# A pipeline over batches from token mixing on, with the feed-forward in four chunks of 386 columns

## The chip, the cores and the metric

The kernel runs on one core of a Trainium2 chip. The metric is the device time of one execution in microseconds (us). The kernel before took 497.8, 505.08 and 505.54 us in three runs, a median of 505.08 us.

## The reference

Three layers run one after another; everything is float32. B = 2, H = 8, S = 768, D = 64, so C = H*D = 512, and F = 1024.

```python
# 1. attention: keep = the first n_global=8 keys, or 0 <= i-j < n_local=96; a bias by distance and head
a = softmax(where(keep, q @ k.T / 8 + bias, -1e9));  x = concat_heads(a @ v)          # [B, S, 512]
# 2. mixing
theta = x @ w_theta                                   # "angles"
zr, zi = x * cos(theta), x * sin(theta)
u = x + w_tok_r @ zr + w_tok_i @ zi                   # token mixing, over S, for each batch
v = u + relu(u @ w_ch)                                # channel mixing
# 3. feed-forward
h = relu(v @ w_in)                                    # [B, S, 1024]
g = h * sigmoid(conv3_over_tokens(h, conv_w))         # tap weights per column, zero padded
out = g @ w_out                                       # [B, S, 512]
```

Token mixing needs all six 128-row tiles of z of its own batch and none of the other batch. The convolution needs one neighbour row on either side.

## The kernel before

Tokens are handled in tiles of 128 rows: NT = 6 per batch, TT = 12 in all. From the angles on, every product is made of three matmuls: each float32 operand is held as a high part (type float32r, made by a copy) and a low part (the float32 value less the high part), and `product` (L373) adds high*high, high*low and low*high into one PSUM bank. So each operand costs a copy, mostly on ACT, and a subtraction, on DVE or POOL. Every engine runs its own list in the order in which it is written; semaphores are the only link between them.

- **Attention** (`banded`, on each engine): 48 units, one for a pair of heads and a tile of queries. PE computes scores, transposed probabilities and the weighted values; ACT takes exponentials and copies; DVE takes maxima (`minus_maxima`, L786), makes the bias tables of the first units (L827) and divides. Meanwhile POOL splits w_theta (L312 and L313), later w_ch and the first rows of w_tok, for which SP issues the loads.
- **Angles** (loops at L493, L635, L932 and L344): for each of 12 tiles PE transposes x and multiplies by w_theta, ACT copies the high part and rounds theta/2pi (L643), DVE makes the low part (L928), reduces the angle in three steps (L938, L942, L945) and clamps it (L948), ACT takes abs, sin and cos (L651, L652, L655), DVE makes x*cos (L957), POOL makes x*sin (L347), ACT copies the high part of both (L661) and POOL makes the two low parts (L351, L353). `r` and the others are double buffered.
- **Token mixing** (L510): 12 groups of 36 matmuls in the order of `MIXES` (L195), both batches side by side, so that each of the six row blocks of w_tok is loaded and split once (`load_w_tok`, L223; `high_rows`, L614; `low_rows`, L918). All of z, for both batches, is 96 KB per partition. DVE adds y to x (L974).
- **Channel mixing** (L525): four chunks of 384 tokens by four blocks of output columns, 12 matmuls each. u is transposed on PE ahead of its use (`transpose_u`, L478), split on ACT (L676) and DVE (L966); v is made on DVE (L994, L1001), copied on ACT (L681) and its low part made on DVE (L981). ACT and POOL split w_in (L696, L358) and w_out (L700, L362) between.
- **Feed-forward** (L542): for each batch, for each of FB = 8 blocks of 128 hidden columns, PE makes h in two halves of 384 tokens (24 matmuls); then relu (L712) and the first tap (L717) on ACT, two taps on DVE (L1017, L1020), sigmoid on ACT (L724), the gate product on DVE (L1027), the high part of g on ACT (L731) and its low part on POOL (L367), all of these over 768 tokens at a time. Behind the eight blocks PE makes the 6 output tiles of the batch, 144 matmuls (L566), ACT copies them out (L750) and SP stores them.

Before the feed-forward of a batch starts, everything ahead of it has ended for both batches. In the feed-forward ACT's and DVE's lists are ordered so:

```python
ACT:  relu(n)  first_tap(n)  sigmoid(n-1)  high_g(n-2)      # relu(n) waits for gate(n-2)
DVE:  conv(n)  gate(n-1)
POOL: low part of g(n-2)
```

Of the kernel before, what the change touches and what calls it, by code (L numbers as in the profile page):

```python
# [29 lines left out]
def build(nc, q, k, v, qk_laid, v_laid, n_global, n_local, w_theta, w_tok, w_ch, w_in, conv_w, w_out, out):  # L30
# [20 lines left out]
    with ctx:  # L51
# [15 lines left out]
        x_flat = x[:].rearrange("p t c -> p (t c)")  # L67
        wch = at("wch", [P, 2, CB, C], F32R, 25)
        wth = at("wth", [P, 2, CB, C], F32R, 41)
        wrows = at("wrows", [P, 2, 2 * NT, P], F32, 57)  # L70
        wraw = at("wraw", [P, CB, C], F32, 69)
        winraw = at("winraw", [P, 2, F], F32, 69)
# [3 lines left out]
        def att(name, shape, dt):  # L76
# [22 lines left out]
        assert a0 <= 207, a0  # L99
# [23 lines left out]
        z = at("z", [P, TT, 2, 2, C], F32R, 77)  # L123
        xT = at("xT", [P, 2, 2, CB * P], F32R, 173)
        th_k = at("th_k", [P, C], F32, 181)
        th_r = at("th_r", [P, 2, C], F32, 183)
        trig = at("trig", [P, 2, 2, C], F32, 187)
        zf = at("zf", [P, 2, 2, C], F32, 69)

        wT = [at("wT0", [P, 2, 2 * NT, P], F32R, 195), at("wT1", [P, 2, 2 * NT, P], F32R, 173)]  # L130

        vT = at("vT", [P, 2, CB, B * S], F32R, 77)
        win = at("win", [P, 2, CB, F], F32R, 125)
        uT = [at("uT0", [P, 2, CB, HALF], F32R, 41), at("uT1", [P, 2, CB, HALF], F32R, 57)]
        vtmp = at("vtmp", [P, 2, HALF], F32, 53)
        g = at("g", [P, 2, FB, S], F32R, 1)
        h_sb = at("h_sb", [P, 2, S + 2], F32, 49)
        cv = at("cv", [P, 2, S], F32, 55.5)
        sg = at("sg", [P, 2, S], F32, 61.5)
        gf = at("gf", [P, 2, S], F32, 67.5)  # L140
        wout = at("wout", [P, 2, FB, C], F32R, 157)
        ob = at("ob", [P, 2, C], F32, 189)
        woutraw = at("woutraw", [P, 4, C], F32, 193)
# [6 lines left out]
            x_all taps_in ident_ready consts_in mask_step bias_ready peak_ready qk_in0 qk_in1 v_in0 v_in1  # L150
            scores_ready max_ready probs_ready pt_ready pt_copied o_ready den_ready rec_ready x_done wraw_in wth_step
            wth_ready wch_ready xt_ready x_hi x_lo theta_ready theta_read k_ready turns_ready r_step r_ready
# [20 lines left out]

        S_BANK = [psum[:, 0:2, :], psum[:, 2:4, :]]
        PT_BANK = [bank[4], bank[5]]
        O_BANK = [bank[6], bank[7]]

        def pair(p):
            return p // HP, 2 * (p % HP)
# [898 lines left out]
```

## Time and profile before

| | |
|---|---|
| median of three runs | 505.08 us (497.8 to 505.54) |
| the profiled execution | 506.55 us, of which its span is 504.8 us |
| PE busy | 439.5 us, 87% of the span |
| DVE, ACT, POOL busy | 281.3, 200.7, 130.5 us |
| granted PE clock, mean | 0.938 of full speed |
| the chain that ended last | PE 55%, DVE 28%, ACT 7%, issue 6%, POOL 2% |
| DMA | 27.46 MB, 54 GB/s over the span |

The span runs from the first to the last instruction of the profiled execution; 1.75 us of that execution's time lie around it. PE's busy time counts matmuls that overlap, so it says where PE had work and not that it ran at its peak. "Granted clock" is the share of full speed that PE's clock was given: 1.00 is 2.4 GHz and 0.50 is 1.2 GHz, and a value between is a mean over a stretch that had both.

### The profile page before, as it was taken

To read this page: it belongs to the slowest core of one execution; us is meant where nothing else is said; L and a number is where in the kernel's file an instruction comes from. 1 tells how busy PE (TensorE), PEld (TensorE's weight loads), DVE (VectorE), ACT (ScalarE), POOL (GpSimd) and SP (SyncE) were. 2 spreads that over 40 slices of the span, in tenths; PEclk is the share of its full clock that TensorE was granted. 3 is DMA by queue.
4 is the path that set the end of the run, shared out by engine and by line. 5 is a ranking of instruction groups with operands and counts; after the bars stand their busy time and mean duration, and the time that the engine had idled before them with its cause. 6 is when DMAs were issued, how large, how long until landed. Compare 5 with 4: busy or idle time off the path is not lost.

```text
span 504.8 us, 6172 instructions
## 1 busy us (share of the span) xinstructions
PE 439.5 (87%) x2352; PEld 374.8 (74%) x2352; DVE 281.3 (56%) x474; ACT 200.7 (40%) x360; POOL 130.5 (26%) x86
## 2 busy tenths in 40 slices
PE   1699999998885677499999999778897999996997
PEld 0488888887764556388888888778897878996875
DVE  5845666669289999502222114879667640266620
ACT  1334666664176656401011003333455541455531
POOL 1500000008037678800000000444413340023340
PEclk9857999998599889889999999889899999999999
DMA  7414333350100000101300002130000002100012
GB/s 288 175 66 130 128 129 130 130 149 16 49 0 1 1 1 1 34 28 64 145 1 0 0 1 83 43 125 1 1 2 0 1 0 83 43 0 1 0 43 84
DMA packets 11119, 27.46 MB, mean 54 GB/s; under 512 B 4176, under 2 KB 4176, under 8 KB 11088
## 3 DMA queue, kind: packets, MB, share of 16 engines
q1 hardware_dynamic: 11088, 27.05, 15.6%
q8 instruction: 19, 0.31, 0.2%
q14 instruction: 12, 0.10, 0.1%
HBM read 23.90 MB, written 3.15 MB: 54 GB/s over the span
## 4 chain that ended last, share of the span: by engine, by line
PE 55%; DVE 28%; ACT 7%; issue 6%; POOL 2%; DMA 1%; DVEq 0%; SPq 0%; ACTq 0%
PE bank L379 27%; PE bank L428 8%; PE bank L566 7%; DVE gf L1027 7%; PE bank L395 6%; PE bank L413 4%; PE bank L400 3%; DVE cv L1017 3%; ACT cv L717 3%; DVE zf L957 3%; ACT h_sb L712 2%; DVE vtmp L1001 2%; DVE th_r L945 2%; DVE th_k L938 1%; DVE th_r L942 1%
## 5 line engine op out<-in xcount | busy, mean ns | idle before, releaser
L379 PE MATMUL bank<-z,wT 128*128 128x512 f32 x432 | 101.9, 397 | 6.9 <-DVE wT L921 6.9
L379 PEld LDWEIGHTS bank<-z,wT 128*128 128x128 f32 x432 | 82.5, 192 | 24.5 <-DVE wT L921 7.3
L379 PE MATMUL bank<-vT,win 128*128 128x384 f32 x384 | 69.7, 341 | 9.7 <-ACT h_sb L712 7.8
L379 PEld LDWEIGHTS bank<-vT,win 128*128 128x128 f32 x384 | 68.0, 192 | 11.3 <-ACT h_sb L712 9.1
L566 PE MATMUL bank<-wout,g 128*128 128x512 f32 x288 | 66.3, 390 | 1.2 <-POOL g L367 1.2
L566 PEld LDWEIGHTS bank<-wout,g 128*128 128x128 f32 x288 | 53.8, 188 | 13.2 <-POOL g L367 2.2
L367 POOL TENSOR_TENSOR g<-gf,g 128x768 fp32r<-128x768 f32 x16 | 34.4, 2154 | 92.4 <-ACT g L731 92.4
L379 PE MATMUL bank<-wth,xT 128*128 128x512 f32 x144 | 42.0, 447 | 18.2 <-DVE xT L928 18.2
L428 PE MATMUL bank<-v_sb,pT 128*128 128x65 f32 x352 | 51.1, 293 | 0.0
L379 PEld LDWEIGHTS bank<-wth,xT 128*128 128x128 f32 x144 | 30.0, 215 | 27.7 <-DVE xT L928 21.2
L428 PEld LDWEIGHTS bank<-v_sb,pT 128*128 128x128 f32 x352 | 49.9, 218 | 0.0
L974 DVE TENSOR_TENSOR x<-bank,x 128x512 f32<-128x512 f32 x12 | 8.3, 690 | 73.5 <-PE bank L379 73.5
L1017 DVE SCALAR_TENSOR_TENSOR cv<-h_sb,convw,cv 128x768 f32<-128x768 f32 x16 | 16.3, 1018 | 55.0 <-ACT cv L717 55.0
L395 PE MATMUL bank<-qk_sb 64*128 64x232 f32 (+1 forms) x192 | 34.6, 442 | 13.4 <-DMA qk_sb<-qk_laid 6.9
L580 ACT ACTIVATE pr<-bank,small 128x232 f32<-128x232 f32 (+1 forms) x96 | 36.7, 437 | 21.4 <-DVE small L786 21.2
L591 ACT ACTIVATE pT<-bank 128x512 f32<-128x512 f32 (+1 forms) x48 | 26.9, 561 | 38.8 <-PE bank L413 38.7
L358 POOL TENSOR_TENSOR win<-winraw,win 128x1024 fp32r<-128x1024 f32 x4 | 9.5, 2380 | 124.9 <-ACT win L696 124.9
L379 PE MATMUL bank<-uT,wch 128*128 128x384 f32 x192 | 38.9, 359 | 1.6 <-DVE vtmp L994 1.6
L379 PEld LDWEIGHTS bank<-uT,wch 128*128 128x128 f32 x192 | 35.7, 202 | 1.9 <-DVE vtmp L994 1.9
L1027 DVE TENSOR_TENSOR gf<-h_sb,sg 128x768 f32<-128x768 f32 x16 | 34.8, 2187 | 0.1
L780 DVE TENSOR_REDUCE small<-bank 128x2 f32<-128x464 f32 (+1 forms) x48 | 29.0, 604 | 10.5 <-PE bank L400 10.5
L712 ACT ACTIVATE h_sb<-bank 128x384 f32<-128x384 f32 x32 | 14.4, 490 | 45.8 <-DVE gf L1027 35.2
(87 smaller groups left out, 546.9 us busy)
## 6 DMA issues: line engine op xcount, KB each, us to landing
qk_sb<-qk_laid SPq DMA_DIRECT2D x8, 792.0 KB, 4.5
v_sb<-v_laid SPq DMA_DIRECT2D x8, 780.0 KB, 4.5
wrows<-w_tok_laid SPq DMA_DIRECT2D x6, 768.0 KB, 4.4
out<-ob SPq DMA_DIRECT2D x12, 256.0 KB, 2.1
winraw<-w_in_in SPq DMA_DIRECT2D x4, 512.0 KB, 4.3
woutraw<-w_out_in SPq DMA_DIRECT2D x8, 256.0 KB, 3.9
wraw<-w_theta_in SPq DMA_DIRECT2D x1, 1024.0 KB, 11.3
wraw<-w_ch_in SPq DMA_DIRECT2D x1, 1024.0 KB, 6.7
```

Of the source, the lines that this page charges most:

```text
L367: pool.tensor_tensor(g[:, 1, n % FB, :], gf[:, n % 2, :], g[:, 0, n % FB, :].bitcast(F32), ALU.subtract)\
L379: last = pe.matmul(dst, w[a], m[b], start=(i == 0 and j == 0), stop=(i == n - 1 and j == 2))
L395: pe.matmul(S_BANK[u % 2][:, h, cols], qk_sb[rows, pp, i * P:(i + 1) * P], qk_sb[rows, pp, S + c0:S + c1], start=True, stop=False)
L413: last = pe.transpose(PT_BANK[u % 2][:, slot * P:(slot + 1) * P], pr[:, u % 2, h, cols], ident[:])
L428: last = pe.matmul(O_BANK[u % 2][:, h * OW:(h + 1) * OW], pT[:, u % 2, slot * P:(slot + 1) * P], v_sb[:, pp, i, chunk, h, :], start=(chunk ...
L566: last = pe.matmul(OUT_BANK[t % 4][:], g[:, hi, f, i * P:(i + 1) * P], wout[:, lo, f, :], start=(f == 0 and j == 0), stop=(f == FB - 1 and ...
L580: last = act.activation(pr[:, u % 2, h, cols], S_BANK[u % 2][:, h, cols], ACT.Exp, bias=small[:, u % 2, 2 + h:3 + h], scale=SCALE)
L591: act.activation(d, src, ACT.Copy).then_inc(pt_copied, 1)
L712: act.activation(h_sb[:, n % 2, 1 + half * HALF:1 + (half + 1) * HALF], H_BANK[n % 2][half][:, 0:HALF], ACT.Relu).then_inc(h_relu, 1)
L780: dve.tensor_reduce(small[:, u % 2, 0:2], S_BANK[u % 2][:, :, cols], AX.X, ALU.max).then_inc(peak_ready, 1)
L1017: dve.scalar_tensor_tensor(out=c, in0=h[:, 1:S + 1], scalar=convw[:, 1, f:f + 1], in1=c, op0=ALU.mult, op1=ALU.add).then_inc(conv_step, 1)
L1027: dve.tensor_tensor(gf[:, m % 2, :], h_sb[:, m % 2, 1:S + 1], sg[:, m % 2, :], ALU.mult).then_inc(g_ready, 1)
```

## The change

The attention's program stays. From the angles on:

- **Angles**: the 12 tiles still come in one row, but sine, cosine and z follow at once only for batch 0 (tiles 0 to 5). Those of batch 1 are made on ACT, DVE and POOL while PE mixes the tokens of batch 0; `th_r` therefore holds six tiles. The clamp moves from DVE to POOL; x*cos and x*sin become one DVE instruction of 1024 columns (`weigh`), the two low parts of z one POOL instruction (`low_z`). PE transposes tile t+1, and ACT and DVE split tile t+2, ahead of the angle of tile t. PE no longer waits for all of x at once.
- **Weights**: POOL splits the first two row blocks of w_tok early instead of w_ch and one block; ACT and POOL split w_ch after the angles. The row blocks of w_tok are loaded and split once for each batch: 12 loads instead of 6.
- **Token and channel mixing**: six groups of batch 0, then those of batch 1 with the channel mixing of batch 0 between them. uT has one buffer instead of two; the low part of v moves from DVE to POOL.
- **Feed-forward**: 4 chunks by 8 blocks, n = 0 to 31, of HC = 386 columns on PE (two of them neighbour rows) and 384 or 386 on the other engines. The first chunk is made between channel-mixing products of batch 1; from then on PE alternates `hidden` of chunk c and `output` of chunk c-1. `ob` has three buffers.

The core of the diff (the lists of PE whole, of the others what the prediction speaks of):

```diff
 @@ SP
-            sp.wait_ge(wth_ready, 1)
-            sp.dma_start(wraw[:], w_ch...)
+            load_w_tok(2)
+            load_w_tok(3)
+            sp.wait_ge(theta_ready, TT)
+            sp.dma_start(wchraw[:], w_ch...)
+            for s in range(4, 9):
+                load_w_tok(s)              # waits for w_lo, s - 3
+            load_w_in(0); load_w_in(1); load_w_tok(9); load_w_in(2)   # load_w_in(c>=2) waits for win_ready
+            load_w_tok(10); load_w_in(3); load_w_tok(11)
 @@ POOL
+            pool.wait_ge(wth_in, 16)
+            pool.tensor_copy(wth[:, 0], wthraw[:]); pool.tensor_tensor(wth[:, 1], ...)
+            for s in range(2):             # the same two for wT[s] from wrows[s]
+            def clamp(t):
+                pool.tensor_scalar(r, r, PI_BELOW, -PI_BELOW, ALU.min, ALU.max).then_inc(r_ready, 1)
+            def low_z(n):
+                pool.tensor_tensor(z[b][:, i, 1], trig[:, n % 2], z[b][:, i, 0]..., ALU.subtract)
+            for t in range(TT):
+                clamp(t)
+                if 2 <= t <= NT + 1:
+                    low_z(t - 2)
+            for n in range(NT, TT):
+                low_z(n)
+            pool.wait_ge(wch_high, 1)
+            pool.tensor_tensor(wch[:, 1], wchraw[:], wch[:, 0]..., ALU.subtract)
 @@ PE
+            x_tile(0)
+            for t in range(TT):
+                if t + 1 < TT:
+                    x_tile(t + 1)
+                theta(t)                   # waits for x_lo of t, and for theta_read of t - 2
+            for s in range(NT):
+                mix_tokens(s)
+            transpose_u(0)
+            mix_tokens(6)
+            mix_channels(0, 0); mix_channels(0, 1); mix_tokens(7); mix_channels(0, 2); mix_channels(0, 3)
+            transpose_u(1)
+            mix_tokens(8)
+            mix_channels(1, 0); mix_channels(1, 1); mix_tokens(9); mix_channels(1, 2); mix_channels(1, 3)
+            transpose_u(2)
+            mix_tokens(10)
+            mix_tokens(11)
+            for j in range(CB):
+                mix_channels(2, j)
+                if j == CB - 1:
+                    transpose_u(3)
+                hidden(j)
+            for j in range(CB):
+                hidden(CB + j)
+                mix_channels(3, j)
+            for c in range(1, NC):
+                for f in range(FB):
+                    hidden(FB * c + f)
+                    output(c - 1, f)       # 9 matmuls; for c - 1 = 0 waits for wout_ready, f + 1
+            for f in range(FB - 2):
+                output(NC - 1, f)
...
 @@ ACT
+            for t in range(TT):
+                turns(t)
+                if t + 2 < TT:
+                    high_x(t + 2)
+                if 1 <= t <= NT:
+                    trigs(t - 1)
+                if 2 <= t <= NT + 1:
+                    high_z(t - 2)
+            for m in range(NT):
+                if m >= 1:
+                    high_rows(m + 1)
+                trigs(NT + m)
+                if m >= 1:
+                    high_z(NT + m - 1)
...
+            def hidden(n):
+                relu(n)                    # waits for h_ready n + 1 and g_ready n - 1
+                first_tap(n)
+                if n >= 1:
+                    sigmoid(n - 1)
+                if n >= 2:
+                    high_g(n - 2)
+            for j in range(CB):
+                hidden(j)
+                high_v(2 * CB + j)
+            high_u(3)
+            for j in range(CB):
+                hidden(CB + j)
+                high_v(3 * CB + j)
+            for c in range(1, NC):
+                for f in range(FB):
+                    if c == 1:
+                        high_w_out(f)
+                    hidden(FB * c + f)
 @@ DVE
+            for t in range(TT):
+                angles(t)
+                if t + 2 < TT:
+                    low_x(t + 2)
+                if 1 <= t <= NT:
+                    weigh(t - 1)
+            for m in range(NT):
+                if m >= 1:
+                    add_y(m - 1)
+                    low_rows(m + 1)
+                weigh(NT + m)
...
+            for j in range(CB):
+                add_mix(2 * CB + j)
+                hidden(j)                  # conv(j), gate(j - 1)
+            low_u(3)
+            for j in range(CB):
+                hidden(CB + j)
+                add_mix(3 * CB + j)
+            for n in range(FB, NH):
+                hidden(n)
```

## Rows read from the trace of the kernel before

**Rows 1.** Busy time by stretch: PE, PEld, DVE, ACT, POOL, clock, DMA, GB/s.
```profile
24.00:42.00 18.00, 18.00 (x84) 14.86 (x84) 8.87 (x33) 6.38 (x17) 0.00 (x0) 0.50 0.24 79
42.00:113.00 71.00, 71.00 (x594) 59.06 (x595) 47.76 (x174) 43.00 (x106) 0.25 (x1) 0.99 0.42 133
113.00:131.00 18.00, 14.35 (x90) 12.97 (x90) 13.30 (x30) 6.18 (x14) 11.03 (x4) 0.74 0.13 45
140.00:197.00 57.00, 39.41 (x166) 30.09 (x166) 54.24 (x62) 37.16 (x59) 39.52 (x27) 0.94 0.00 1
212.00:306.00 94.00, 93.89 (x408) 77.16 (x408) 16.74 (x20) 7.80 (x8) 1.18 (x1) 0.97 0.10 37
306.00:357.00 51.00, 41.41 (x229) 39.89 (x228) 40.65 (x57) 21.18 (x39) 18.93 (x11) 0.93 0.19 62
```

**Rows 2.** PE's timeline: start, duration, operation, count, idle before and its releaser.
```profile
126.05 3.51 PE L428 MATMUL bank<-v_sb,pT 128*128 128x65 f32 x16
133.34 5.49 PE L379 MATMUL bank<-wth,xT 128*128 128x512 f32 x12 [0.62 <-DVE xT L928]
196.91 8.32 PE L379 MATMUL bank<-z,wT 128*128 128x512 f32 x36
212.11 14.04 PEld L379 LDWEIGHTS bank<-z,wT 128*128 128x128 f32 x52 [7.30 <-DVE wT L921]
316.54 0.82 PE L485 MATMUL bank<-ident,x 128*128 128x128 f32 x6
361.83 22.00 PE L379 MATMUL bank<-vT,win 128*128 128x384 f32 x126
413.67 16.63 PE L566 MATMUL bank<-wout,g 128*128 128x512 f32 x72 [0.57 <-POOL g L367]
484.98 16.66 PE L566 MATMUL bank<-wout,g 128*128 128x512 f32 x72 [0.60 <-POOL g L367]
```

**Rows 3.** Timeline of the feed-forward and the channel mixing: ACT, POOL and DVE.
```profile
378.38 0.87 ACT L712 ACTIVATE h_sb<-bank 128x384 f32<-128x384 f32 x2 [3.20 <-DVE gf L1027]
384.87 0.87 ACT L712 ACTIVATE h_sb<-bank 128x384 f32<-128x384 f32 x2 [3.18 <-DVE gf L1027]
388.26 2.25 POOL L367 TENSOR_TENSOR g<-gf,g 128x768 fp32r<-128x768 f32 x1 [4.24 <-ACT g L731]
388.73 2.58 DVE L1027 TENSOR_TENSOR gf<-h_sb,sg 128x768 f32<-128x768 f32 x1
310.40 0.56 DVE L1001 TENSOR_TENSOR vtmp<-vtmp,uT 128x384 f32<-128x384 f32 x1
```

**Rows 4.** Groups by line and shape: busy us, mean ns, idle before.
```profile
L957 DVE TENSOR_TENSOR zf<-x,trig 128x512 f32<-128x512 f32 x12 | 15.7, 1312 | 0.9 <-ACT trig L655 0.7
L948 DVE TENSOR_SCALAR th_r<-th_r 128x512 f32<-128x512 f32 x12 | 14.8, 1230 | 0.4
L358 POOL TENSOR_TENSOR win<-winraw,win 128x1024 fp32r<-128x1024 f32 x4 | 9.5, 2380 | 124.9 <-ACT win L696 124.9
L681 ACT ACTIVATE vT<-vtmp 128x384 fp32r<-128x384 f32 x16 | 8.4, 525 | 21.6 <-DVE vtmp L1001 21.6
```

**Rows 5.** DVE's timeline of the angles: ten L938, first and last; one L957.
```profile
147.01 0.91 DVE L938 TENSOR_SCALAR th_k<-th_k 128x512 f32<-128x512 f32 x1
199.57 0.41 DVE L938 TENSOR_SCALAR th_k<-th_k 128x512 f32<-128x512 f32 x1
158.19 0.68 DVE L957 TENSOR_TENSOR zf<-x,trig 128x512 f32<-128x512 f32 x1
```

**Rows 6.** Timeline of POOL and DVE at the start and end of attention.
```profile
15.41 1.89 POOL L312 CAST wth<-wraw 128x2048 fp32r<-128x2048 f32 x1 [12.52 <-DMA wraw<-w_theta_in]
17.23 4.90 DVE L827 SCALAR_TENSOR_TENSOR bias<-mb,ma 128x232 bf16<-128x232 f32 x2
115.84 3.43 DVE L786 TENSOR_SCALAR small<-small 128x2 f32<-128x2 f32 x1
```

**Rows 7.** The page's list of DMA issues: KB each, median us to landing.
```profile
wrows<-w_tok_laid SPq DMA_DIRECT2D x6, 768.0 KB, 4.4
```

More of the change, by code:

```diff
@@ new lines, in output @@
+            def output(c, f, tiles=(0, 1, 2)):
+                if f == 0:
+                    if c == 0:
+                        pe.wait_ge(u_lo, NC * CB)
+                    if c <= 1:
+                        pe.wait_ge(r_done, NC * CB)
+                    if c >= 2:
+                        pe.wait_ge(out_copied, 3 * (c - 1))
+                if c == 0:
+                    pe.wait_ge(wout_ready, f + 1)
+                pe.wait_ge(g_lo, FB * c + f + 1)
+                for i in tiles:
+                    for j, (hi, lo) in enumerate(((0, 0), (0, 1), (1, 0))):
+                        last = pe.matmul(OUT_BANK[c % 2][i][:], g[c % 2][:, hi, f, i * P:(i + 1) * P], wout[:, lo, f, :],
+                                         start=(f == 0 and j == 0), stop=(f == FB - 1 and j == 2))
+                    if f == FB - 1:
+                        last.then_inc(out_ready, 1)
@@ L572, in _ @@
+            for i in range(3):
+                output(NC - 1, FB - 2, (i,))
+                output(NC - 1, FB - 1, (i,))
         @block.scalar
@@ L686, in _, with high_w_in @@
+            def high_w_in(c):
                 if c == 0:
[L687 to L700 removed]
@@ L707, in relu @@
+            high_rows(7)
+            high_u(0)
+            high_w_in(0)
+            high_rows(8)
+            high_v(0)
+            high_v(1)
+            high_w_in(1)
+            high_rows(9)
+            high_v(2)
+            high_v(3)
+            high_u(1)
+            high_w_in(2)
+            high_rows(10)
+            high_v(4)
+            high_v(5)
+            high_w_in(3)
+            high_rows(11)
+            high_v(6)
+            high_v(7)
+            high_u(2)
             def relu(n):
+                half = n // FB % 2
+                act.wait_ge(h_ready, n + 1)
@@ new lines, in _ @@
+            add_y(5)
+            low_rows(7)
+            low_u(0)
+            add_y(6)
+            low_rows(8)
+            add_mix(0)
+            add_mix(1)
+            add_y(7)
+            low_rows(9)
+            add_mix(2)
+            add_mix(3)
+            low_u(1)
+            add_y(8)
+            low_rows(10)
+            add_mix(4)
+            add_mix(5)
+            add_y(9)
+            low_rows(11)
+            add_mix(6)
+            add_mix(7)
+            low_u(2)
+            add_y(10)
```

739 lines of the change are left out of this document (346 added, 393 removed).

## The prediction, made before the changed kernel was run

> **What bounds it now.** I read first the busy time by stretch, then PE's timeline at the borders of the stages, then the order in which ACT, DVE and POOL end each other's waits. PE bounds token mixing alone, where it is busy for 93.89 of 94 us and DVE for 17 [rows 1]. In the angles it is DVE's and POOL's turn: PE works 39 of 57 us, DVE 54. In channel mixing PE works 41 of 51 us. In the feed-forward relu(n) on ACT is idle 3.2 us for the gate product of two blocks earlier, and the blocks come every 384.87 - 378.38 = 6.49 us [rows 3], while PE needs 24 matmuls at 22.00/126 = 0.175 us, 4.2 us [rows 2]. In attention the clock is 0.50 for 18 us near the start and 0.74 near the end [rows 1], both behind a stall of DVE [rows 6].
>
> **PE's work behind the angles.** It hardly changes, so the stage is costed as work plus stalls. A matmul of 512 columns costs (16.66 - 0.23)/72 = 0.228 us, where 0.23 is my allowance for the last one's drain; one of 384 columns 0.175 us, of 386 0.176 [rows 2]. Token mixing 432 x 0.228 = 98.5; output 288 x 0.228 = 65.7; channel mixing 192 x 0.175 = 33.6; hidden 384 x 0.176 = 67.5; transposes 48 x 0.82/6 = 6.6. Sum 271.9 us. Before, the first token matmul starts at 196.91 and the last output matmul ends at 484.98 + 16.66 = 501.64: 304.7 us, so about 33 us are not work. One stall is in plain sight: 7.30 us for the second row block [rows 2].
>
> **Is PE fed in the new feed-forward?** With chunk c's hidden and chunk c-1's output, PE needs 12 x 0.176 + 9 x 0.228 = 4.16 us a step. The other engines' ring is: relu, tap, sigmoid, high part, each 0.525 at this width [rows 4], so POOL starts at 2.1; POOL takes half of 2.25 and ends at 3.2; the gate product, queued on DVE behind the two taps and held until POOL ends, adds 0.56 [rows 3]: 3.8 us. The same ring at full width gives the 6.49 that is measured: POOL ends at 388.26 + 2.25 = 390.51 and the gate at 391.31 [rows 3]. So PE bounds, with 0.4 us to spare. The first chunk runs beside channel mixing: PE 12 x 0.351 = 4.2; DVE five instructions of 0.56, 2.8; ACT five, 2.6. POOL there has the low parts of g and of v, about 1.05 each; DVE's gate, two taps and vtmp take turns with it: 4 x 0.56 + 2.1 = 4.3. I charge 0.3 x 8 = 2.4 us. What is queued behind the new waits: high_u(3) stands on ACT behind hidden(3) and one high_v, and uT now has one buffer; I find u's low part ready 8.4 us after the last product of chunk 2, where PE has work for 5.8: 3 us. The first output waits for w_out's split, which ACT starts behind hidden(7) and high_v(15) and POOL ends: 2 us. w_ch's low part on POOL (twice the 2.38 of 1024 columns [rows 4]) holds low_rows(7) on DVE, and low_u(0) behind it, just until mixing group 6 ends: 2 us. Sum 9.4, say 10. Hence 282 us for 304.7: -23.
>
> **What hides the rest.** Six more row blocks of w_tok are loads of 4.4 us [rows 7] on an SP queue where a load is due every 8.2 us or more; the next row block needs about 1.5 + 2.7 us of ACT and DVE, inside a group's 8.2. load_w_tok(10) is queued behind load_w_in(2), which waits for POOL, but is needed two groups later. Batch 1's sine, weigh and low_z (ACT 3, DVE 1.2, POOL 2.4 per tile) are beside 8.2 us of PE. The third buffer of ob only shortens a wait before the tail; the tail's 3.2 us from 501.64 to the end I leave.
>
> **Angles.** Before, ten of the reductions start from 147.01 to 199.57, 5.84 us apart [rows 5]. The row that explains it: the 512-column product on DVE takes 0.68 alone [rows 5] and 1.31 in the mean, the clamp 1.23 in the mean [rows 4], and the feed-forward's gate 2.58 beside POOL [rows 3]. So instructions with two SBUF inputs, or the clamp's kind, wait for POOL. Per tile DVE has 0.41 + 0.68 + 0.41 + 0.68 = 2.2 of these and POOL three of about 1.2: together 5.8. After: DVE 0.41 + 0.68 + 1.16 (1024 columns, by the slope between 0.56 for 384 and 0.68 for 512) = 2.25; POOL low_z 2.38 and the clamp. The clamp on POOL is in no row: below, the cast's rate, 1.89/4 = 0.47; above, the two-input 1.2. I take 0.65, nearer the cast, which has one input too. Period 5.3 (5.1 to 5.8) for the six tiles of batch 0; then four tiles without sine. From the first angle matmul to the third reduction were 147.01 - 133.34 = 13.7, of which 2.8 for the cold clock (5.49 for 12 matmuls against 2.7): 10.9. Then 6 x 5.3 = 31.8, and 8 for the last two products with their waits: 50.7 to the first token matmul. Before 196.91 - 133.34 = 63.6. So -13.
>
> The Trainium skill (GPSIMD Engine Reference, Key points) says that GpSimd shares its SBUF interfaces with VectorE, to the cost of DVE instructions in a two-port mode or with two SBUF inputs. The trace agrees (0.68 against 1.31). Without that rule the period would be ACT's own, near 4.2, and the result 7 us lower.
>
> **Attention.** Its program stays, but POOL's work beside it moves. Removed near the end: w_ch's and the first row block's split, which held DVE for 3.43 us at 115.84 [rows 6] and cooled the clock. The 90 matmuls from 113 would take 90/8.37 = 10.8 us at the rate of 594 in 71 us [rows 1], ending at 124 to 126, not at 126.05 + 3.51 = 129.56: -4. Added near the start: two row blocks behind w_theta's split, 2 x 0.75 x (1.89 + 4.6) = 9.7 us of POOL, where 4.6 is what held DVE at 17.23 [rows 6]. It prolongs the stall and the 18 us at clock 0.50, which did 84 matmuls where 10 us would do. At least 3 (one stall), at most 10 (two stalls and 9 more cold us); I take 5, near the lower end, since DVE gets its turns between POOL's instructions and PE is cold there anyway. Net +1. The start of the angles loses its wait for all of x: 3.8 us from 129.56 to 133.34 become 2.7: -1.
>
> **Sum.** -23 - 13 + 1 - 1 = -36 from the profiled execution's 506.55 (504.8 of span and 1.75 around it), 471 in rounding; that execution lies 1.5 above the median of 505.08, which is inside the spread of the three runs, so I forecast 471 us.
>
> **Rivals.**
> *A, the ring is slower than PE.* Twice as many instructions, each with a fixed share (0.56 for 384 columns against 0.68 for 512 is 0.2 of it), and turns with POOL for the taps as well. For it: 0.4 us of slack is little, and in chunk 1 POOL splits w_out besides. Against: the full-width ring comes out exactly. At 4.8 us a step, 32 steps: +20, 491.
> The Trainium skill (VectorE: DVE Perf Modes, The TRN2 errata) speaks against this change: the fixed cost falls between instructions, so tiles should have 512 elements or more. The rows above show the fixed share; a change cut to its rule would have kept 768 columns. It comes to rival A's time.
> *B, the angles gain nothing.* The clamp on POOL queues behind low_z and delays sine, and the start of attention costs its upper end: 5.84 us a tile as before, 484.
> *C, order without overlap.* Single uT, ACT's order and the later splits bring back stalls like the 33 us that are there now: 494 and up to 500.
> *D, slower.* The ring is a latency, not a rate: relu(n+1) behind gate(n-1), in turn behind POOL's low part. Were a half-width block to take 6.49 as a full one does, 32 of them take 208 us against 133: 546. From 4.16 + 36/32 = 5.3 us a step nothing is left, from 5.6 it is slower by 2%. Against it: every row of ACT and DVE scales with width but for 0.2 us.
>
> **Chances.** Forecast 0.60 (457 to 481 by itself), A 0.15, B 0.09, C 0.08, D 0.06, better than 457 by 0.02. Range: low, 10 of the terms' bounds less and 4 fewer stalls, 457; high 494, which takes in A and B and the start of C. A measurement of this kernel tells about 2% from no change: faster needs less than 495. So faster 0.86, within 2% 0.08, slower 0.06.
>
> **What would show it.** Token mixing starts near 184 and PE is nearly solid from there, its clock near 1.00; hidden steps 4.2 us apart with a gate that still waits for POOL; angles 5.3 apart for six tiles; the end of attention near 131 with the cold stretch longer than before and no stall near 115. Wrong if steps stand over 4.6 apart, if PE idles for low_u, or if attention ends beyond 137.

## The result and the profile after

The changed kernel takes 475.3 us (median of four runs, 469.75 to 475.82); the kernel before, with one more run beside them, 502.18 (497.8 to 505.54). The ratio is 0.947 (95%: 0.934 to 0.959). The forecast was 471, the range 457 to 494. The profiled execution took 475.66 us, 473.9 of them its span.

The page after: busy time, and the chain that ended last.
```profile
PE 429.0 (91%) x2352; PEld 368.4 (78%) x2352; DVE 274.7 (58%) x498; ACT 215.0 (45%) x414; POOL 142.4 (30%) x107
PE 76%; DVE 15%; ACT 3%; POOL 3%; issue 2%; DMA 1%; DVEq 0%; SPq 0%; ACTq 0%
```
The chain is 76% PE where it was 55%: the angles and some stops excepted, most of the kernel now runs at PE's pace.

Busy time by stretch after, with the columns of [rows 1]: two of attention, angles, token mixing with what lies beside it, chunk 0 of the feed-forward, chunk 1, the rest.
```profile
24.00:32.00 8.00, 3.85 (x18) 3.10 (x18) 7.96 (x6) 0.79 (x2) 7.92 (x3) 0.75 0.30 101
113.00:131.00 18.00, 16.87 (x144) 14.70 (x145) 11.97 (x44) 10.14 (x24) 0.00 (x0) 1.00 0.22 85
140.00:183.00 43.00, 33.20 (x142) 25.80 (x140) 39.75 (x41) 23.97 (x40) 22.36 (x15) 0.92 0.00 1
183.00:301.00 118.00, 118.00 (x562) 101.00 (x561) 51.61 (x59) 45.70 (x60) 40.44 (x21) 1.00 0.24 81
301.00:344.00 43.00, 39.87 (x221) 39.04 (x219) 25.54 (x43) 20.08 (x41) 12.91 (x12) 0.96 0.08 25
344.00:388.00 44.00, 35.72 (x160) 30.94 (x161) 21.80 (x28) 20.09 (x41) 23.76 (x18) 0.92 0.09 24
388.00:471.00 83.00, 82.79 (x406) 73.74 (x404) 42.08 (x50) 38.28 (x79) 23.14 (x19) 1.00 0.09 33
```
From 183 to 301 PE is never idle and its clock is 1.00; before, only token mixing was nearly so, with a clock of 0.97, and channel mixing had 10 idle us [rows 1]. Behind 183, the two stretches that are not full are 301 to 344 and 344 to 388.

PE's timeline after, at the borders of the stages and in chunk 1.
```profile
126.62 1.96 PE L462 MATMUL bank<-v_sb,pT 128*128 128x65 f32 x16
130.58 3.01 PE L413 MATMUL bank<-wth,xT 128*128 128x512 f32 x12 [1.13 <-DVE xT L920]
156.21 3.02 PE L413 MATMUL bank<-wth,xT 128*128 128x512 f32 x12 [0.70 <-DVE xT L920]
161.96 3.06 PE L413 MATMUL bank<-wth,xT 128*128 128x512 f32 x12 [2.30 <-DVE xT L920]
182.98 49.13 PE L541 MATMUL bank<-z,wT 128*128 128x512 f32 x216
324.97 3.90 PE L413 MATMUL bank<-uT,wch 128*128 128x384 f32 x12 [2.75 <-DVE uT L1075]
341.32 2.30 PE L413 MATMUL bank<-vT,win 128*128 128x386 f32 x12
350.11 4.18 PE L596 MATMUL bank<-wout,g 128*128 128x512 f32 x9 [6.50 <-POOL wout L380]
362.07 2.33 PE L596 MATMUL bank<-wout,g 128*128 128x512 f32 x9 [0.73 <-POOL wout L380]
404.07 2.27 PE L413 MATMUL bank<-vT,win 128*128 128x386 f32 x12
408.24 2.27 PE L413 MATMUL bank<-vT,win 128*128 128x386 f32 x12
452.26 18.53 PE L596 MATMUL bank<-wout,g 128*128 128x512 f32 x81
```
These answer to [rows 2]. By them each term of the sum can be set against the run:

| part of the span | before | forecast | measured |
|---|---|---|---|
| attention, to its last matmul | 129.6 | 130.6 | 128.6 |
| to the first angle matmul | 3.8 | 2.7 | 2.0 |
| angles, to the first token matmul | 63.6 | 50.7 | 52.4 |
| from there to the last output matmul | 304.7 | 282 | 287.8 |
| tail | 3.2 | 3.2 | 3.1 |

The gain is 11 us in the angles and 17 us behind them. With the 1.0 and 1.8 us ahead of the angles it is the 31 us between the two profiled executions (506.55 and 475.66); between the medians it is 27, since the profiled execution of the kernel before was longer than its median. The hidden steps stand 408.24 - 404.07 = 4.17 us apart, where 4.16 was worked out.

### The profile page after: what moved, and what is told of

Same layout as the page of the kernel before. It is cut to its first block, busy times and chain, and to the rows that moved or that the text cites. A ratio compares the mean times of both kernels' runs of the same rounds, so it can differ in the third digit from the quotient of the medians.

```text
span 473.9 us, 6319 instructions
## 1 busy us (share of the span) xinstructions
PE 429.0 (91%) x2352; PEld 368.4 (78%) x2352; DVE 274.7 (58%) x498; ACT 215.0 (45%) x414; POOL 142.4 (30%) x107
## 4 chain that ended last, share of the span: by engine, by line
PE 76%; DVE 15%; ACT 3%; POOL 3%; issue 2%; DMA 1%; DVEq 0%; SPq 0%; ACTq 0%
PE bank L541 21%; PE bank L413 20%; PE bank L596 13%; PE bank L462 8%; PE bank L429 6%; PE bank L447 4%; PE bank L434 3%; DVE th_k L926 3%; DVE bias L952 2%; DVE trig L1044 1%; POOL wout L380 1%; DVE th_r L933 1%; PE bank L552 1%; DVE xT L920 1%; DVE small L893 1%
## 5 line engine op out<-in xcount | busy, mean ns | idle before, releaser
L596 PE MATMUL bank<-wout,g 128*128 128x512 f32 x288 | 72.1, 400 | 8.7 <-POOL wout L380 8.7
L413 PE MATMUL bank<-vT,win 128*128 128x386 f32 x384 | 73.9, 342 | 0.0
L386 POOL TENSOR_TENSOR g<-gf,g 128x384 fp32r<-128x384 f32 x32 | 38.9, 1218 | 65.5 <-ACT g L821 65.5
L1122 DVE SCALAR_TENSOR_TENSOR cv<-h_sb,convw,cv 128x384 f32<-128x384 f32 x32 | 21.9, 685 | 59.7 <-ACT cv L805 59.7
L799 ACT ACTIVATE h_sb<-bank 128x386 f32<-128x386 f32 x32 | 15.8, 492 | 79.4 <-PE bank L413 79.4
L413 PE MATMUL bank<-wth,xT 128*128 128x512 f32 x144 | 39.1, 426 | 10.9 <-DVE xT L920 10.9
L462 PE MATMUL bank<-v_sb,pT 128*128 128x65 f32 x352 | 48.1, 282 | 0.0
L347 POOL TENSOR_SCALAR th_r<-th_r 128x512 f32<-128x512 f32 x12 | 8.3, 691 | 127.9 <-DVE th_r L933 127.9
L352 POOL TENSOR_TENSOR z<-trig,z 128x1024 fp32r<-128x1024 f32 x12 | 32.3, 2697 | 32.5 <-ACT z L721 32.5
L375 POOL TENSOR_TENSOR vT<-vtmp,vT 128x384 fp32r<-128x384 f32 x16 | 17.9, 1127 | 74.5 <-ACT vT L758 74.5
```

The lines of the kernel that those rows point to most:

```text
L352: pool.tensor_tensor(z[b][:, i, 1], trig[:, n % 2], z[b][:, i, 0].bitcast(F32), ALU.subtract)\
L375: pool.tensor_tensor(vT[b][:, 1, j, cols], vtmp[:, n % 2, :], vT[b][:, 0, j, cols].bitcast(F32), ALU.subtract).then_inc(v_lo, 1)
L386: pool.tensor_tensor(g[c % 2][:, 1, f, :], gf[:, n % 2, :], g[c % 2][:, 0, f, :].bitcast(F32), ALU.subtract).then_inc(g_lo, 1)
L413: last = pe.matmul(dst, w[a], m[b], start=(i == 0 and j == 0), stop=(i == n - 1 and j == 2))
L462: last = pe.matmul(O_BANK[u % 2][:, h * OW:(h + 1) * OW], pT[:, u % 2, slot * P:(slot + 1) * P], v_sb[:, pp, i, chunk, h, :], start=(chunk ...
L596: last = pe.matmul(OUT_BANK[c % 2][i][:], g[c % 2][:, hi, f, i * P:(i + 1) * P], wout[:, lo, f, :], start=(f == 0 and j == 0), stop=(f == ...
```

## The experiments

Times are medians; each run is set against the changed kernel's 475.3. The kernel before took 502.7 to 505.1 in the medians beside them, and 502.2 beside the changed kernel, so a difference of under 3 us is not told from none. Traces differ too: in the nine traces that have the changed kernel's attention word for word (its own, ff_blocks, ff_ring, mix_blocks, clamp_dve, turns_act, order3, late_out, relu_first) attention's last matmul ends at 124.4 to 131.3 us, with 128.5 in the middle. What follows therefore compares stretches of a trace from their own start. The diffs are excerpts; `...` marks what is left out.

**ff_blocks: no alternation on PE.**
```diff
                 for f in range(FB):
                     hidden(FB * c + f)
+                for f in range(FB):
                     output(c - 1, f)
```


> The changed kernel, but in chunks 1 to 3 PE makes all eight hidden blocks of a chunk and then all eight output steps of the chunk before, instead of one by one. My theory (PE is fed only because 2.05 us of output stand between two hidden blocks, so that a step is longer than the other engines' ring of 3.8 us): the hidden blocks of a chunk then come at the ring's pace, about 27 us instead of 17, and the outputs add 16.4 us as before; +10 us for each of three chunks, about 505. Rival (the gain of the feed-forward is that of shorter chunks, whose ring ends beside the outputs whatever their order): within 5 us of the changed kernel, 471 to 480.

487.4 us (ratio to before 0.967, 0.957 to 0.976), +12. PE's timeline in chunk 2:
```profile
383.68 6.51 PE L413 MATMUL bank<-vT,win 128*128 128x386 f32 x36
401.81 2.39 PE L413 MATMUL bank<-vT,win 128*128 128x386 f32 x12 [1.43 <-ACT h_sb L800]
405.63 2.38 PE L413 MATMUL bank<-vT,win 128*128 128x386 f32 x12 [1.43 <-ACT h_sb L800]
407.85 16.51 PE L596 MATMUL bank<-wout,g 128*128 128x512 f32 x72
```
Hidden blocks come 405.63 - 401.81 = 3.82 us apart, at the ring's pace, and PE waits for relu each time. The mechanism is the theory's; my size was not: eight blocks took 407.85 - 383.68 = 24.2 us, not 27, since the first three come without a wait, so a chunk costs 40.5 for 33.4 (8 x 4.17), 7 more. Chunk 1 gains 3.6 us, because its first output no longer waits for w_out.

**ff_ring: PE's bound taken away.** Of the output's three products only high*high is made, 3 matmuls a step for 9.

```diff
-                    for j, (hi, lo) in enumerate(((0, 0), (0, 1), (1, 0))):
-                        last = pe.matmul(OUT_BANK[c % 2][i][:], g[c % 2][:, hi, f, ...], wout[:, lo, f, :], ...
+                    last = pe.matmul(OUT_BANK[c % 2][i][:], g[c % 2][:, 0, f, ...], wout[:, 0, f, :], ...
```


> The changed kernel with only the high*high product of the output, 3 matmuls a step instead of 9 (the two other products are left out). It takes PE's bound away from the ring. My theory (ring 3.8 us, PE 4.17): hidden blocks come 3.7 to 3.9 us apart in chunks 2 and 3; the total falls by 24 steps x 0.4 and by 48 matmuls x 0.228 behind the last step, about 20 us, to 455. Rival (the ring itself is at 4.17 or over and PE only follows): blocks stay 4.17 or more apart and the total falls by 11, to 464.

454.3 us (0.901, 0.893 to 0.909), -21. PE in chunk 2:
```profile
399.61 2.39 PE L413 MATMUL bank<-vT,win 128*128 128x386 f32 x12 [0.75 <-ACT h_sb L798]
403.45 2.39 PE L413 MATMUL bank<-vT,win 128*128 128x386 f32 x12 [0.75 <-ACT h_sb L798]
```
3.84 us between these two, 3.83 in the mean of the ten steps from 395.79 to 434.10: the ring, measured by itself, against 3.8 worked out from rows at full width. Rival A is refuted for chunks 2 and 3: there the ring has 0.34 us to spare under PE's 4.17.

**mix_blocks: no overlap within mixing.**
```diff
-            transpose_u(0); mix_tokens(6); mix_channels(0, 0); mix_channels(0, 1); mix_tokens(7); ...
+            for s in range(NT, TT):
+                mix_tokens(s)
+            transpose_u(0); mix_channels(0, 0..3); transpose_u(1); mix_channels(1, 0..3); transpose_u(2)
```


> The changed kernel without the overlap inside mixing: PE makes the six token groups of batch 1 in one row, then the channel mixing of batch 0, with ACT's, DVE's and SP's lists in the same order. My theory: the single buffer of uT then shows three times (transposes, four copies, four low parts, about 4 us each, with a colder clock behind), and channel mixing alone runs at DVE's and POOL's pace, 2.5 us a product instead of 2.1: +15 to +18 us, about 492. Rival (the overlap of mixing is worth nothing, the gain is in the angles and the feed-forward): within 4 us of the changed kernel.

ACT's and DVE's lists and SP's loads follow the same order. 484.1 us (0.960, 0.951 to 0.969), +9, half of the theory's size. PE waits for uT (1.68 us, 3.41 and 3.42 by its timeline; behind two of these its clock falls, and twelve matmuls took 3.78 us for 2.26), but the products themselves stay at 2.1 us: the split of uT is what the overlap hides, and DVE and POOL keep up with channel mixing alone, which I had doubted.

**clamp_dve: the clamp back on DVE.**
```diff
-                pool.tensor_scalar(r, r, PI_BELOW, -PI_BELOW, ALU.min, ALU.max).then_inc(r_ready, 1)
+                dve.wait_ge(r_step, t + 1)        # at the end of angles(t)
+                dve.tensor_scalar(r, r, PI_BELOW, -PI_BELOW, ALU.min, ALU.max).then_inc(r_ready, 1)
```


> The changed kernel with the clamp of the angles back on DVE. The angle products of the middle tiles came 5.8 us apart, where I had expected 5.3. Theory 1 (DVE's and POOL's instructions that share the SBUF interface add up): POOL loses 0.69 a tile and DVE gains 0.41, 5.5 us apart, total -2 us. Theory 2 (what costs is the clamp's place on POOL behind the low part of z, which makes the sine late): 4.3 to 4.8 apart, total -6 to -9 us. Theory 3 (DVE's own list bounds): 6.3 or more apart, total +3 us or more.

476.9 us (0.948, 0.939 to 0.956), +1.6, not to be told from none. Its angles take 126.39 to 182.82, 56.4 us, where the traces with the changed kernel's angles have 52.4 to 53.8; its attention happened to end 4 us earlier. Products of the middle tiles are 161.04 - 155.03 = 6.0 apart. Nearest is theory 3, at half its size. DVE's timeline in the changed kernel, then here:
```profile
157.25 2.61 DVE L926 TENSOR_SCALAR th_k<-th_k 128x512 f32<-128x512 f32 x1
```
```profile
156.04 0.41 DVE L925 TENSOR_SCALAR th_k<-th_k 128x512 f32<-128x512 f32 x1
157.93 2.45 DVE L935 TENSOR_SCALAR th_r<-th_r 128x512 f32<-128x512 f32 x1
160.91 1.21 DVE L1045 TENSOR_TENSOR trig<-trig,x 128x1024 f32<-128x1024 f32 x1
```
The same subtraction takes 2.61 or 0.41: in each of these two kernels one DVE instruction a tile waits out POOL's low part of z, and those behind it in DVE's list stand in its queue. What sets the pace is seen on ACT and POOL. In the changed kernel:
```profile
159.67 0.63 ACT L711 ACTIVATE trig<-th_r 128x512 f32<-128x512 f32 x1 [2.08 <-POOL z L352]
161.34 1.04 ACT L721 ACTIVATE z<-trig 128x1024 fp32r<-128x1024 f32 x1
162.46 2.89 POOL L352 TENSOR_TENSOR z<-trig,z 128x1024 fp32r<-128x1024 f32 x1 [0.45 <-ACT z L721]
165.44 0.63 ACT L711 ACTIVATE trig<-th_r 128x512 f32<-128x512 f32 x1 [2.09 <-POOL z L352]
```
This is a ring through the two buffers of `trig`: abs and sine of a tile, then in ACT's list z's high part of the tile before, then its low part on POOL, for which the next abs waits. It closes in 165.44 - 159.67 = 5.77 us, the period. With the clamp on DVE the sine waits for the clamp instead, which ends 0.28 us behind POOL's low part (157.93 + 2.45 = 160.38 against 157.29 + 2.81 = 160.10): the ring with that step in it is the 6.0.

**turns_act: th_k's subtraction on ACT.**
```diff
-                dve.tensor_scalar(turns, turns, ROUND, None, ALU.subtract).then_inc(turns_ready, 1)
+                act.wait_ge(k_ready, t + 1)       # behind turns(t)
+                act.activation(th_k[:, t % 2, :], th_k[:, t % 2, :], ACT.Copy, bias=-ROUND).then_inc(turns_ready, 1)
```


> The changed kernel with the subtraction that ends the rounding of theta/2pi (th_k, 0.41 us on DVE) made by ACT instead. Theory (the angles' period of 5.8 us is DVE's own list, 3.7, plus one instruction, this one, that waits for nearly all of POOL's low part of z): DVE gets to its PSUM-reading step while POOL runs, and only the rest of POOL's time is waited for: 4.3 to 4.9 us apart in the middle tiles, total -5 to -8 us. Rival 1 (only the sum of the time on the shared interface counts): 5.4 apart, -2 us. Rival 2 (ACT bounds): no change.

472.5 us (0.933, 0.927 to 0.939), -2.8, not to be told from none in the total; but the angles, 133.31 to 183.20, are 49.9 us for 52.4, and 5.36 a tile. The waiting subtraction is gone, yet the size is rival 1's:
```profile
154.08 2.47 POOL L352 TENSOR_TENSOR z<-trig,z 128x1024 fp32r<-128x1024 f32 x1 [1.64 <-ACT z L723]
155.18 0.69 DVE L930 SCALAR_TENSOR_TENSOR th_r<-th_k,bank 128x512 f32<-128x512 f32 x1 [0.87 <-ACT th_k L676]
156.64 0.63 ACT L713 ACTIVATE trig<-th_r 128x512 f32<-128x512 f32 x1 [1.01 <-POOL z L352]
```
DVE's step that reads PSUM now runs beside POOL in its usual 0.69 us, as the theory had it. The ring through `trig` is still there and still closes the period: the next abs starts at 162.00, 5.36 later. It is 0.4 us shorter than in the changed kernel because POOL's low part takes 2.47 us for 2.89; there `weigh` came late on DVE, behind the subtraction, and the two ran at the same time for 0.6 us, here for 0.2. That is read from the traces and was not tested by itself.

**late_splits: the two row blocks of w_tok split behind the angles' busy tiles.**
```diff
+                if t == NT + 1:                   # in POOL's loop over t; wT[0]
+                    split_rows(0)
+            split_rows(1)                         # behind the loop
```


> The changed kernel with POOL's splits of the first two row blocks of w_tok moved out of the start of attention, one behind the low part of z of tile 5 and one behind the last clamp. Theory (they hold DVE and so PE at the start, and lengthen the stretch at clock 0.50): the stall of PE at 28 us goes, attention ends about 5 us earlier, near 123.5; in the angles they hold DVE's reductions of tiles 9 to 11 for 2 to 4 us; together -1 to -3 us against the changed kernel. Rival (DVE has its turns between POOL's instructions, the start costs nothing): attention ends where it did, and the total is 2 to 4 us higher.

474.2 us (0.938, 0.934 to 0.943), -1.1, not to be told from none. Both halves are there in the traces: attention ends at 122.25 for 128.58, and the angles take 124.25 to 179.41, 55.2 us for 52.4, with 1.10 more before the second group. The three traces without the early splits and with w_theta's split whole (this, best and best_z) end attention at 122.25, 123.27 and 123.32, the nine with them at 124.4 to 131.3: the early splits cost some 5 us at the start, by the middle values, and the single traces leave 1 to 9. PE at the start in the changed kernel:
```profile
24.36 0.97 PE L429 MATMUL bank<-qk_sb 64*128 64x232 f32 x4 [3.88 <-ACT pr L649]
33.03 0.80 PE L429 MATMUL bank<-qk_sb 64*128 64x128 f32 x4 [4.83 <-ACT pr L649]
```
The second stop is the splits'; the first is that of the kernel before (3.32 us there).

**order3: three lists reordered where the feed-forward starts.**
```diff
 ACT, from hidden(4) on
-                hidden(CB + j); high_v(3 * CB + j)
+                hidden(CB + j)
+                if j >= 1: high_v(3 * CB + j - 1)         # the last behind hidden(8)
-                high_w_out(f); hidden(FB * c + f)
+                hidden(FB * c + f); high_w_out(f)
 POOL, low_v one block later too
-                low_w_out(f); low_g(FB - 2 + f)
+                low_w_out(f); low_g(FB - 1 + f)
 ACT and DVE
+                if j == CB - 1: high_u(3)                 # low_u(3) on DVE; ahead of hidden(3)
 PE
-                    hidden(FB * c + f); output(c - 1, f)
+            for n in range(FB, NH):
+                hidden(n)
+                if n >= FB + 2: output((n - 2) // FB - 1, (n - 2) % FB)
 ... the last two of these outputs behind the loop; ACT copies outputs out two blocks later too
```


> The changed kernel with another order at the start of the feed-forward: v's high part stands on ACT one block later, so relu(n+1) no longer stands behind channel mixing's last product; PE makes the output of a block two blocks later; u's split of the last chunk goes ahead of hidden(3) on ACT and DVE. Theory (the first output waited 6.5 us because ACT's order let the ring fall 3 us behind PE and w_out's split follows it; channel mixing of chunk 3 waited 2.75 for uT behind hidden(3)): the wait before the first output is gone, that for uT is 1 us or less, the 0.7 us waits of chunk 1 go too; -9 to -12 us, about 465. Rival (the ring is slow there because POOL makes two low parts and DVE five steps): the ring still takes 5 us a step, PE waits elsewhere for it, -3 to -5 us.

462.1 us (0.914, 0.910 to 0.918), -13. PE waits 1.86 before the first output and for nothing else between 285 and 460. Two more runs take the edits apart; the earlier split of uT was not run alone.

**late_out: PE's order alone.**

```diff
-                    hidden(FB * c + f); output(c - 1, f)
+            for n in range(FB, NH):
+                hidden(n)
+                if n >= FB + 2: output((n - 2) // FB - 1, (n - 2) % FB)
 ... and ACT's copies of the outputs
```


> The changed kernel with PE's order alone changed: it makes the output of a block two blocks later (and ACT copies chunks out two blocks later). ACT's, DVE's and POOL's orders around v, and uT's split, are as in the changed kernel. Theory A (the wait before the first output is w_out's split being late, and PE only lacked other work): PE fills it with hidden 9 and 10, the wait falls from 6.5 to 2.5 us or less and the 0.7 us waits of chunk 1 go, since w_out's low part is then two blocks ahead; -7 to -9 us against the changed kernel, about 467. Theory B (the ring, 3 us behind PE from chunk 0's second half, is the cause): PE then waits for relu instead, about as long, and the gain is 3 us or less.

466.1 us (0.922, 0.914 to 0.929), -9: theory A. PE:
```profile
325.81 3.10 PE L413 MATMUL bank<-uT,wch 128*128 128x384 f32 x12 [2.74 <-DVE uT L1077]
347.78 2.38 PE L413 MATMUL bank<-vT,win 128*128 128x386 f32 x12 [1.18 <-ACT h_sb L801]
350.70 2.32 PE L596 MATMUL bank<-wout,g 128*128 128x512 f32 x9 [0.54 <-POOL wout L380]
```
6.50 becomes 1.18 + 0.54; the wait for uT stands as it was. ACT in its chunk 1:
```profile
356.08 0.49 ACT L801 ACTIVATE h_sb<-bank 128x386 f32<-128x386 f32 x1 [1.34 <-DVE gf L1135]
359.91 0.49 ACT L801 ACTIVATE h_sb<-bank 128x386 f32<-128x386 f32 x1 [1.34 <-DVE gf L1135]
```
Here the ring catches up with PE while w_out is being split, and its pace is 359.91 - 356.08 = 3.83 us: w_out's split does not lengthen it, so rival A is refuted for chunk 1 as well. order3 is 4.0 us faster than this run and does not have its wait for uT (2.74 us, and 0.9 more in the cold matmuls behind it).

**relu_first: ACT's and POOL's order alone.**

```diff
 ACT
-                high_v(3 * CB + j)                        # behind hidden(CB + j)
+                if j >= 1: high_v(3 * CB + j - 1)
-                high_w_out(f); hidden(FB * c + f)
+                hidden(FB * c + f); high_w_out(f)
 POOL
-                low_w_out(f); low_g(FB - 2 + f)
+                low_w_out(f); low_g(FB - 1 + f)
```


> The changed kernel with the first of order3's edits alone: in the second half of chunk 0 v's high part stands on ACT one block later, and POOL's list follows. PE's order and uT's split are left. Theory (ACT's order alone made the ring 5.2 us a step there): relu comes at PE's 4.2 us, the first output waits 3 us or less (w_out's split, which starts on ACT behind the last v) instead of 6.5; -4 to -6 us. Rival (late output order did the work in order3): -1 us or less.

522.3 us (1.041, 1.031 to 1.051), +47; both of its runs lie above every run of the kernel before. Neither theory has room for that. relu does come at PE's pace now, 4.21 us apart from 331.26 to 343.90, but the first output still waits 6.08, and in chunk 1 a step takes 11.3 us in the mean (10.7 to 12.1). PE, ACT and POOL by the timeline:
```profile
398.68 3.14 PE L417 MATMUL bank<-vT,win 128*128 128x386 f32 x12
406.74 4.20 PE L600 MATMUL bank<-wout,g 128*128 128x512 f32 x9 [4.92 <-POOL wout L380]
401.85 0.49 ACT L803 ACTIVATE h_sb<-bank 128x386 f32<-128x386 f32 x1 [9.58 <-PE bank L417]
403.89 1.26 POOL L386 TENSOR_TENSOR g<-gf,g 128x384 fp32r<-128x384 f32 x1 [9.28 <-ACT g L825]
405.11 1.57 POOL L380 TENSOR_TENSOR wout<-woutraw,wout 128x512 fp32r<-128x512 f32 x1
```
For the output of a step, w_out's high part on ACT now stands behind the same step's relu, and its low part on POOL behind the low part of g that comes with that relu: hidden block (to 401.82), relu, sigmoid and g on ACT, POOL twice, output at 406.74, one after another, and the next hidden block only behind that. Either place is enough for it: w_out's high part ends at 403.72 + 0.61 = 404.33, so with POOL's order restored its low part could start 0.8 us earlier at most. It is rival D's kind of loss, a ring that no longer overlaps; in the changed kernel w_out is one block ahead in both lists, and no more. order3 has the same two lists and does not suffer, because its outputs come two blocks later. The parts of order3 are not additive: the reorder on ACT and POOL loses 47 us alone, and beside PE's later outputs it costs nothing that can be seen (PE waits 1.86 us before the first output there, 1.72 in late_out).

**best, best_z, best_zp.** best is order3, turns_act and late_splits together; best_z has high_z ahead of trigs on ACT in the angles; best_zp also splits w_theta in pieces at the start of attention.
```diff
 best_zp, POOL
-            pool.tensor_copy(wth[:, 0], wthraw[:]) ... pool.tensor_tensor(wth[:, 1], wthraw[:], ...)
+            for q in range(8):                    # the same two for 256 columns each
```
```diff
 best_z, ACT in the angles; high_z(t - 2) under its own condition
-                trigs(t - 1); high_z(t - 2)
+                high_z(t - 2); trigs(t - 1)
```


> late_splits, turns_act and order3 together. Theory (three separate stretches of time): their gains add up, 20 us or so under the changed kernel, about 455. Rival (POOL's moved splits and the quicker angles collide in tiles 8 to 11): 3 to 5 us less than the sum.

> best with z's high part ahead of the next sine on ACT in the angles. In turns_act the middle tiles came 5.36 apart, and ACT's abs waited 1.0 for POOL's low part of z two tiles earlier, which itself had waited behind the next tile's sine. Theory (a ring through the two buffers of trig: two tiles in 10.7 us): with the copy 1.8 us earlier the ring opens and the period falls to 4.6 to 5.0, ACT's and DVE's own; -2 to -4 us against best. Rival (the interface is the bound, 5.3 in all): no change.

> best_z with w_theta's split at the start of attention in eight pieces of 256 columns. Theory (what stops PE at 20 us is one POOL instruction of 4.6 us that DVE's must wait out, and the clock of 0.50 over the following 18 us comes from that stop): DVE waits 0.6 us at a time, PE is never idle for 2 us, its clock stays near 1.00, attention ends 6 to 10 us earlier; -6 to -10 us against best_z. Rival (DVE gets one instruction between POOL's, so that the same 6.5 us are lost in pieces): PE stops in pieces, the clock falls all the same, within 2 us of best_z.

best 457.4 us (0.906, 0.903 to 0.910), best_z 459.8 (0.913, 0.904 to 0.921), best_zp 447.3 (0.891, 0.886 to 0.896). The three gains, 13.2, 2.8 and 1.1, sum to 17.1, and best has 17.9: the medians add up, though two of the three are within the spread. best_z is no better: its tiles are 5.47 apart, and its weigh now waits:
```profile
156.86 2.69 DVE L1057 TENSOR_TENSOR trig<-trig,x 128x1024 f32<-128x1024 f32 x1 [0.85 <-ACT trig L726]
156.07 2.40 POOL L352 TENSOR_TENSOR z<-trig,z 128x1024 fp32r<-128x1024 f32 x1
```
The copy ahead of the sine opens the ring through `trig`, as the theory had it, but closes another: weigh, which has two SBUF inputs, now starts inside POOL's low part and takes 2.69 us for 1.2; z's high part waits for weigh, abs, sine and cosine stand behind it on ACT, and the next weigh waits for the cosine. So the ring of trig was the bound at 5.36 a tile, and this one stands right behind it at 5.47. In best_zp the stop that every other trace has shortly behind 20 us is gone, by stretch:
```profile
24.00:32.00 8.00, 7.99 (x66) 6.50 (x66) 7.18 (x26) 5.28 (x14) 1.42 (x3) 1.00 0.32 108
```
66 matmuls from 24 to 32 us at clock 1.00, where the kernel before did 40 and the changed one 18. The first angle matmul comes at 112.72 instead of best_z's 125.33. It is the fastest version, 28 us under the changed kernel.

## Why the prediction was right, step by step

The profiled execution is 4.7 us over the 471: 5.8 and 1.7 behind and in the angles, less 2.7 in attention and at its border and 0.1 in the tail. So errors of both signs met in the total.

**PE's work, 271.9 us, and the step of 4.16.** Right: the pace is 4.17, and ff_ring measured the ring that had to fit under it at 3.83. The ring could be foretold because the same chain of ends gives the full-width block's 6.49. Its terms were a little off and cancel: POOL's low part takes 1.28 us (1.1 taken), and the gate ends 0.41 behind it (0.56 taken). ff_blocks shows that the alternation carries it. No run keeps blocks of 768 columns and alternates, so what the narrower blocks do by themselves is not shown.

**Stalls behind the angles, 10 us.** Too small: 287.8 - 271.9 = 15.9. Two of its terms did not come, POOL beside the first chunk (2.4) and w_ch's low part (2): PE has no wait from 183 to 322. The other two, 5 us, became 17, with PE's work about 1 us less than costed. The wait for uT was costed at 3 and is 2.75, with 1.7 more in the cold matmuls behind it. The first output was costed at 2; it waited 6.50, its nine matmuls took 4.18 for 2.2 and the next block 3.02 for 2.3: 9 us. The step that failed is the second half of the chunk beside channel mixing. I had compared DVE's, ACT's and POOL's sums with PE's 4.2 and found 4.3. But the lists close a ring there. ACT and DVE in the changed kernel:
```profile
336.91 1.41 DVE L1122 SCALAR_TENSOR_TENSOR cv<-h_sb,convw,cv 128x384 f32<-128x384 f32 x1 [1.62 <-ACT cv L805]
339.94 0.56 DVE L1086 TENSOR_TENSOR vtmp<-vtmp,uT 128x384 f32<-128x384 f32 x1
340.54 0.53 ACT L758 ACTIVATE vT<-vtmp 128x384 fp32r<-128x384 f32 x1 [2.84 <-DVE vtmp L1086]
345.77 0.52 ACT L758 ACTIVATE vT<-vtmp 128x384 fp32r<-128x384 f32 x1 [2.85 <-DVE vtmp L1086]
346.20 0.61 ACT L771 ACTIVATE wout<-woutraw 128x512 fp32r<-128x512 f32 x1
```
v's high part stands on ACT ahead of relu; DVE's first tap waits for ACT's and takes 1.41 us beside POOL's low part of v (0.62 without it); second tap, gate and channel mixing's sum follow in DVE's list, and the next high part waits for that sum. The ring closes in 345.77 - 340.54 = 5.23 us, with ACT idle for 2.8 of them, while PE's products come every 4.2. w_out's split starts at 346.20, behind the last of these, where PE had come for it at 341.32 + 2.1 = 343.4, and POOL has two low parts to make first. Which of the two, ACT's chain or w_out's place behind it, costs more is left open: relu_first takes the ring away but puts w_out's split one place later on both lists, and the wait stays at 6.08; late_out mends neither, PE fills the wait, and 1.72 is left; order3 has relu_first's lists and late_out's order on PE, and 1.86 is left. Three waits of 0.7 in chunk 1 came too, for w_out on POOL; with the blocks around them they are 3.4 us that I had not charged. The prediction called it a sign of being wrong if PE idled for low_u. It did, for 2.75 us, and the sum had charged 3 for it: that sign was badly chosen.

**Angles, 50.7 us.** 52.4. The clamp on POOL takes 0.61 alone (0.65 taken) and 0.69 in the mean. Period 5.75 where 5.3 was forecast, 2.7 us over six tiles; the rest came out 1.0 better. The step that failed in size is the period as a sum of the time that both engines want the interface for, and the old kernel's agreement (5.8 against 5.84) was partly luck. What counts in the changed kernel is the ring through `trig`, 5.77, in which POOL's low part takes 2.89 us where it runs partly beside weigh and 2.40 where it starts alone. The per-tile pace is thus hardly better than before; the gain is that only six tiles pay it. By clamp_dve the move of the clamp is worth 2.6 to 4 us of the 11; the rest, from the six tiles that need no sine in the row, is argued and not shown, since no run put sine and cosine of batch 1 back.

**Attention, +1.** -1 in the profiled execution, and with a spread of 7 us between like traces that agreement is luck as much as reckoning. late_splits, best and best_z have the start of the kernel before and no POOL at the end: attention ends at 122.25 to 123.32 where it was 129.56, so the end was worth 6 to 7 us (4 forecast), and the early splits cost about 5 (5 forecast).

**The rivals.** A is refuted by ff_ring for chunks 2 and 3 and by late_out for chunk 1. The steps of chunk 1 do come (387.37 - 354.09)/7 = 4.75 us apart in the changed kernel, over the 4.6 that was named as a sign, but for want of w_out one block earlier and not of the ring. The Trainium skill (VectorE: DVE Perf Modes, The TRN2 errata) asks for tiles of 512 elements or more. The traces have a cost of that kind: two rings of 3.83 for 768 columns against one of 6.49, 1.2 us more. But that time lies under PE's 4.17 a step in chunks 2 and 3, so it costs nothing there. B did not happen in its time, though the period came nearly to its 5.84. Its 484 is 471 and the 13 of the angles alone; with the upper end of attention's start, which it names too, it would have been 489. C is seen in two places, 2.75 and 6.50 us, not in 33. D did not happen; relu_first shows how near it stood.

The Trainium skill (GPSIMD Engine Reference, Key points) names the shared interface. The traces read here agree that DVE's instructions with two SBUF inputs (weigh, 1.2 against 2.69 us), or of the kind of th_k's subtraction (0.41 against 2.61), wait beside POOL. What my use of it missed is that the wait falls on one instruction and on all behind it in the list, and that it counts only where it lies on the ring.

## What to carry to other kernels

Work out the ring of the engines that feed PE from the rows at the present width, check that it gives the present period, and only then scale it; compare it with PE's own step with the filler in between. At the seams between stages sums per engine are not enough: follow which list stands behind which wait, and by how many blocks a producer is ahead, since one block less made this kernel 47 us slower. Where PE waited for one late product here, giving it two blocks of other work gained 9 us, and reordering the producers' lists did not. Where several lists meet, look for every ring, also of copies through two buffers: opening the one of 5.36 us only laid bare one of 5.47.

## What the runs showed of the hardware that was not expected

A single POOL instruction can cost more than its own length on the other engines. In best_z w_theta's low part is one instruction of 4.6 us, from 17.35 to 21.95. DVE's two bias instructions, 0.59 us together where POOL is idle (at 23.36), wait for it:
```profile
17.20 4.91 DVE L965 SCALAR_TENSOR_TENSOR bias<-mb,ma 128x232 bf16<-128x232 f32 x2
```
PE stops at 20.4 us for 3.3, and its clock, 0.95 in the mean from 12 to 24 us, is granted at 0.50 (1.2 GHz) from 24 to 42. With the same work in sixteen instructions of 0.4 to 1.0 us, PE is busy 11.63 of the 12 us from 12 to 24 and the clock stays at 1.00: 12.6 us earlier at the first angle matmul, and 12.4 in the medians, from moving no work at all. In the changed kernel a second stop, 4.83 us at 28, comes behind the first, and the clock is 0.50 until 48 and 0.98 from 48 to 60. The spread of attention goes with that cold stretch: in the nine traces with the same attention the clock's mean from 42 to 60 us lies between 0.66, where attention ends last (131.3), and 1.00, in the three where it ends before 126.
